# One-hot rows of the slot tables laid out two tiles side by side instead of eight, in a recurrence with two expert layers

## What is computed

```python
# x, f_logit: (2, 5056, 256); N = 10112 tokens, D = 256, E = 8 experts, F = 1024
f = lower_bound + (1 - lower_bound) * sigmoid(f_logit)
for t in range(S):
    h = f[:, t] * h + (1 - f[:, t]) * x[:, t];  y[:, t] = h
x = y.reshape(N, D)
# layer 0: router by cosine similarity over tau; layer 1: router by x @ w_gate
expert_idx = argmax(logits, axis=1)
gate_w = softmax(logits)[arange(N), expert_idx]
for e in range(E):
    mask = expert_idx == e
    out[mask] = gate_w[mask, None] * (relu(x[mask] @ w1[e]) @ w2[e])
```

## Time and profile before

| | |
|---|---|
| Median of 3 runs | 1358.53 us (1357.48 to 1358.74) |
| The profiled execution, its own time | 1355.69 us |
| Its span, first to last instruction | 1353.9 us |
| Busy: PE / PEld | 98% / 94% |
| Busy: DVE / ACT / POOL | 72% / 61% / 32% |
| Mean granted clock of PE | 0.984 |

### The profile page before, as it was taken

The page is one execution under the profiler, slowest core; times in us unless marked ns, Lnnn a source line. Parts: engine busy times, 40 slices in busy tenths (PEclk is TensorE's granted clock), DMA queues, the critical chain, the costliest instruction groups (busy, mean ns, idle before and its releaser), DMA issues.

```text
span 1353.9 us, 30681 instructions
## 1 busy us (share of the span) xinstructions
PE 1324.5 (98%) x10645; PEld 1266.2 (94%) x10645; DVE 974.0 (72%) x1471; ACT 825.6 (61%) x1390; POOL 427.3 (32%) x459
## 2 busy tenths in 40 slices
PE   7999989999999999999999999999999999999996
PEld 6995449999999999999999999899999999999996
DVE  5877337777777777789877789777777777777773
ACT  5775246666666666666656666556666666666662
POOL 5663012111111111123222243224444444444432
PEclk9998699999999999999999999999999999999998
DMA  7999528666677666679767667447666666666650
GB/s 272 334 319 307 2 91 293 215 227 213 221 230 231 213 226 214 220 235 164 235 212 221 232 194 229 157 156 233 221 214 222 229 222 203 222 226 224 219 179 1
DMA packets 205671, 287.00 MB, mean 212 GB/s; under 512 B 41270, under 2 KB 167876, under 8 KB 205604
## 3 DMA queue, kind: packets, MB, share of 16 engines
q1 hardware_dynamic: 192068, 250.90, 59.8%
q0 software_dynamic: 13536, 35.21, 7.8%
HBM read 252.59 MB, written 35.44 MB: 213 GB/s over the span
## 4 chain that ended last, share of the span: by engine, by line
PE 93%; DVE 3%; ACT 1%; POOL 1%; issue 1%; DMA 0%; DVEq 0%; SPq 0%; ACTq 0%; POOLq 0%
PE bank L1522 39%; PE bank L1502 39%; PE bank L1426 4%; PE bank L1486 3%; PE bank L1402 2%; PE bank L1388 1%; PE bank L1367 1%; PE bank L1348 1%; PE bank L1361 1%; DVE hT L453 1%; DVE gx L443 1%; POOL fg L994 1%; DMA w1raw<-in_moe_w 0%; ACT th L1186 0%; ACT sq L1200 0%
## 5 line engine op out<-in xcount | busy, mean ns | idle before, releaser
L1502 PE MATMUL bank<-xs,w1h 128*128 128x256 f32 x3008 | 558.4, 283 | 3.0 <-DVE hl L743 1.5
L1502 PEld LDWEIGHTS bank<-xs,w1h 128*128 128x128 f32 x3008 | 460.7, 188 | 4.6 <-DVE hl L743 1.7
L1269 ACT ACTIVATE hh<-bank 128x512 fp32r<-128x512 f32 x376 | 224.6, 597 | 388.7 <-PE bank L1502 388.7
L1522 PE MATMUL bank<-w2h,hl 128*128 128x264 f32 (+1 forms) x1504 | 424.9, 282 | 0.0
L1522 PE MATMUL bank<-w2h,hh 128*128 128x264 f32 (+1 forms) x1504 | 424.9, 282 | 0.0
L1522 PE MATMUL bank<-w2l,hh 128*128 128x264 f32 (+1 forms) x1504 | 424.6, 282 | 0.0
L1502 PE MATMUL bank<-xs,w1l 128*128 128x256 f32 x1504 | 419.9, 279 | 0.0
L743 DVE SCALAR_TENSOR_TENSOR hl<-bank,hh 128x512 fp32r<-128x512 f32 x376 | 259.9, 691 | 189.0 <-ACT hh L1269 185.1
L1522 PEld LDWEIGHTS bank<-w2l,hh 128*128 128x128 f32 x1504 | 283.3, 188 | 0.0
L1522 PEld LDWEIGHTS bank<-w2h,hh 128*128 128x128 f32 x1504 | 283.2, 188 | 0.0
L1522 PEld LDWEIGHTS bank<-w2h,hl 128*128 128x128 f32 x1504 | 282.9, 188 | 0.0
(11 more groups left out here) (172 smaller groups left out, 960.4 us busy)
## 6 DMA issues: line engine op xcount, KB each, us to landing
w1raw<-in_moe_w SPq DMA_DIRECT2D x94, 1024.0 KB
w2raw<-in_moe_w SPq DMA_DIRECT2D x94, 1024.0 KB, 5.6
rows_b<-yb SPq DMA_DIRECT2D x94, 128.0 KB, 2.2
xin<-in_x SPq DMA_DIRECT2D x19, 512.0 KB, 5.2
fin<-in_f_logit SPq DMA_DIRECT2D x19, 512.0 KB, 7.0
rows_a<-h_rows SPq DMA_DIRECT2D x19, 512.0 KB, 5.3
w_stage<-in_moe_w SPq DMA_DIRECT2D x12, 512.0 KB, 7.9
xb<-rows_a,row_i POOLq DMA_INDIRECT x94, 4.9
```

The lines of the kernel that those rows point to most:

```text
L1269: nc.scalar.activation(hh[:, j, :], bank[j % UB][:, :], ACT.Relu).then_inc(hid_hi, 1)
L1502: ins = mm(bank[j % UB][:, f * GW:(f + 1) * GW], w[p][:, o:o + P], xs[:, p, a, c * GW:(c + 1) * GW], start=k == 0, stop=k == 3 * DC - 1)
L1522: ins = mm(bank[Y_BANK + rows_slot(i, t)][:, 0:n], a[:, j, f * GW + t * P:f * GW + (t + 1) * P], w[p][:, 2 * j + f, 0:n], start=(j, f, k) ...
```

## The change

`lane_oh`, `tile_oh` and `vals` get the layout [partition, chunk slot, pair of tiles, lane or slot tile, 2]: two tiles lie side by side instead of eight, and the four pairs of a chunk follow each other. TensorE reads both operands with a step of two elements, 4 bytes. The tables of numbers are repeated twice instead of eight times, and read again for each pair. VectorE's three operations now have rows of two elements innermost. Where a chunk has an odd number of tiles (the last of table 0, seven) the row is filled up; the column of `where` behind the last tile gets -1 from a GpSimd memset, for which VectorE's wait on `rep_ok` goes from 2 to 3. The number of instructions of each engine in a chunk stays, and so do the orders of work.

```diff
+        RH = RC // 2
-        lane_oh = sb("lane_oh", [P, RS, P, RC], bf16, sr)
-        tile_oh = sb("tile_oh", [P, RS, ST, RC], bf16, sr)
-        vals = sb("vals", [P, RS, 2 * ST, RC], bf16, sr)
+        lane_oh = sb("lane_oh", [P, RS, RH, P, 2], bf16, sr)
+        tile_oh = sb("tile_oh", [P, RS, RH, ST, 2], bf16, sr)
+        vals = sb("vals", [P, RS, RH, 2 * ST, 2], bf16, sr)
...
-        lane_rep = sb("lane_rep", [P, P, RC], bf16, sr)
-        tile_rep = sb("tile_rep", [P, ST, RC], bf16, sr)
+        lane_rep = sb("lane_rep", [P, P, 2], bf16, sr)
+        tile_rep = sb("tile_rep", [P, ST, 2], bf16, sr)
...
-                dve.wait_ge(rep_ok, 2)
+                dve.wait_ge(rep_ok, 3)
...
-                v.tensor_tensor(tile_oh[:, g % RS, 0:W, 0:w], tile_rep[:, 0:W, 0:w],
-                                where[:, 0, t0:t0 + w].unsqueeze(1).to_broadcast([P, W, w]),
-                                ALU.is_equal).then_inc(oh_ok, 1)
-                v.tensor_tensor(lane_oh[:, g % RS, :, 0:w], lane_rep[:, :, 0:w],
-                                where[:, 1, t0:t0 + w].unsqueeze(1).to_broadcast([P, P, w]),
-                                ALU.is_equal).then_inc(lane_ok, 1)
+                h = -(-w // 2)
+                def of_two(ap2, n):
+                    return ap2.rearrange("p (h r) -> p h r", r=2).unsqueeze(2).to_broadcast([P, h, n, 2])
+                v.tensor_tensor(tile_oh[:, g % RS, 0:h, 0:W, :],
+                                tile_rep[:, 0:W, :].unsqueeze(1).to_broadcast([P, h, W, 2]),
+                                of_two(where[:, 0, t0:t0 + 2 * h], W), ALU.is_equal).then_inc(oh_ok, 1)
+                v.tensor_tensor(lane_oh[:, g % RS, 0:h, :, :],
+                                lane_rep[:, :, :].unsqueeze(1).to_broadcast([P, h, P, 2]),
+                                of_two(where[:, 1, t0:t0 + 2 * h], P), ALU.is_equal).then_inc(lane_ok, 1)
                 dve.wait_ge(oh_ok, g + 1)
-                v.tensor_tensor(vals[:, g % RS, 0:W, 0:w], tile_oh[:, g % RS, 0:W, 0:w],
-                                tileno[:, t0:t0 + w].unsqueeze(1).to_broadcast([P, W, w]),
-                                ALU.mult).then_inc(valt_ok, 1)
+                v.tensor_tensor(vals[:, g % RS, 0:h, 0:W, :], tile_oh[:, g % RS, 0:h, 0:W, :],
+                                of_two(tileno[:, t0:t0 + 2 * h], W), ALU.mult).then_inc(valt_ok, 1)
...
-                    pool.iota(table[:, :, :], pattern=[[1, count_t], [0, RC]], base=0,
+                    pool.iota(table[:, :, :], pattern=[[1, count_t], [0, 2]], base=0,
...
+                pool.memset(where[:, :, TT:TT + 1], -1.0).then_inc(rep_ok, 1)
...
-                nc.scalar.activation(vals[:, g % RS, W:2 * W, 0:w], tile_oh[:, g % RS, 0:W, 0:w],
+                h = -(-w // 2)
+                nc.scalar.activation(vals[:, g % RS, 0:h, W:2 * W, :], tile_oh[:, g % RS, 0:h, 0:W, :],
                                      ACT.Copy, scale=part1[:, 0:1]).then_inc(valp_ok, 1)
...
-                    ins = mm(table, lane_oh[:, g % RS, :, t], vals[:, g % RS, 0:2 * W, t],
+                    ins = mm(table, lane_oh[:, g % RS, t // 2, :, t % 2],
+                             vals[:, g % RS, t // 2, 0:2 * W, t % 2],
                              start=first and t == 0, stop=last and t == w - 1)
```

## The result

| | before | after |
|---|---|---|
| Median | 1358.01 us (1356.64 to 1358.74) | 1315.51 us (1315.29 to 1316.71) |
| The profiled execution | 1355.69 us | 1315.59 us |
| Its span | 1353.9 us | 1313.8 us |
| Mean granted clock | 0.984 | 0.993 |

The ratio is 0.969 (95% interval 0.9677 to 0.9702): 42.5 us faster. The forecast was 36.3 us and 1322; the result lies 1.5 us under 1317, the low end of the range given. The two profiled executions differ by 40.1 us, the rest is that the one of before was a quick one of its kind, so 40.1 is what can be laid out by place.

A forecast was written before the change was run, and what follows sets the result against it. TensorE was taken to bound the kernel, 91% of the span. Gains of 23.0 (table 0) + 13.0 - 1.4 (table 2) + 1.7 (table 1) = 36.3 us, off the median 1358.53, gave 1322.2; range 1317 to 1332.

The forecast's parts named there:

- the step isn't the cause: Rival: L1426 is slow for another reason, TensorE keeps 0.34 and 0.231 us, time 1358.5; 3%.
- The walk: Table 0 followed chunk by chunk through TensorE, VectorE and ScalarE: stage ends at 150.1, not 173.16, 23.0 us earlier.
- The clock's rival: Rival: TensorE's clock still falls in table 0, gate steps 6.5 us longer, gain 28, time 1330.2; 6%.
- I take the middle, 0.093, for all three widths: TensorE's new pace at L1426: 0.093 us a matmul with 188, 124 or 64 columns, between 0.08 and 0.106.
- The upper bound, 0.106: TensorE's slowest expected pace, from sixteen eight-column matmuls in 1.69 us, each loading 128 fp32 weights 4 bytes apart.
- the 256-column row: Up block's twelve fp32r matmuls in 1.42 us: 256 columns 4 bytes apart take 0.118 us, 0.46 ns a column.
- the 1.7 of the sum: Table 1's term: 64 matmuls going from 0.120 to 0.093 us, 1.7 us gained.
- the lower bound of 0.08: TensorE's fastest expected pace, 0.08 us, from a bf16 matmul with 188 columns at a step of 2 bytes.
- a stretch in which VectorE was near full: From 832, VectorE busy 13.20 of 14.00, loads idle 0.69 us; charged to table 2's four steps, 1.4 us taken.
- the cliff I gave 7%: Rival: VectorE falls to one element a cycle on rows of two, time 1341.6; 7%.
- The slower rival: Rival: VectorE walks short rows one by one, 5 ns a place, table 0 20 us late, time 1402; 3%.
- the forecast's best case of 39.9: Sum of the three tables' gains at 0.08 us a matmul and no stall: 23.1 + 14.2 + 2.6 us.

The follow-up runs named there:

- weights_only: Against the kernel before, only the weights (lane_oh) get pairs side by side, tile_oh and vals keep eight; 1354.43 us, ratio 0.9982.
- moving_only: Against the kernel before, only the moving operand (tile_oh and vals) gets pairs side by side, the weights keep a step of 16 bytes; 1319.8 us.
- four_side: Against the changed kernel, four tiles side by side in place of two, a step of 8 bytes for both operands; 1323.81 us.
- lag: The changed kernel with TensorE's chunks of tables 1 and 2 one tick later than VectorE's; 1311.82 us.
- one_side: Against the changed kernel, one tile by itself, both TensorE operands contiguous, VectorE's innermost rows of one element; 1340.65 us.

## Why the prediction was off, point by point

- **The mechanism was right.** TensorE's table matmuls were slow for the step of their operands and for nothing else (`weights_only`, `moving_only`, `four_side`); the rival "the step isn't the cause" is out.
- **Table 0: right in kind and size.** 23.5 us against 23.0. The walk gave chunks 0 to 5 at VectorE's pace, 6 to 8 at ScalarE's, the end at 150.1; with the start 0.8 earlier it came at 148.8. The pace that was wrong below is worth 0.7 us at most on the 79 matmuls here (0.093 less 0.084 each), and the waits for VectorE and ScalarE hid a part of it. The clock's rival didn't happen (its 6.5 us for three gate steps should have been 7.1 by its own rows, 15.7 less 3 x 2.89). L556 (now L557) waits 3.35 us, foretold as about 4.
- **The step that failed: "I take the middle, 0.093, for all three widths, since the narrow ones would be held by the load."** Measured: 0.084 for 188 columns, 0.056 for 124 and 0.030 for 64. The upper bound, 0.106, came from a load of 128 fp32 weights; a bf16 load isn't like it, it takes 0.060 even at 16 bytes (`moving_only`) and 0.030 or less at 4. I had the moving pace, 0.46 ns a column, in hand from the 256-column row: by it alone table 1 comes to 0.029 and table 2 to 0.057. Table 1 gave 5.3 us, three times the 1.7 of the sum and twice its best bound of 2.6, since the lower bound of 0.08 was itself for 188 columns and couldn't bound 64.
- **Table 2: two errors that partly cancel, so that 11.6 against 10.8 is in part luck.** TensorE's own step is 13.28 (`lag`) and not 13.8; over the table its matmuls alone were worth 15.4 us (80.33 less 64.96) and not 13.0. But the loop over three engines took 1.2 us a step (14.46 against 13.28), and not 0.35: I had charged the idle time of a stretch in which VectorE was near full, and no wait of one engine for the next in a circle. The step came to 14.46, foretold 14.2. The step in which the first chunk falls, where the chain runs over VectorE's preparation of the table, gave 0.6 us back; I had nothing there.
- **VectorE's rows of two: right.** 684 and 544 ns. `one_side` shows that the cliff I gave 7% is real and lies one step further, at 25 us.
- **The slower rival** had the right threshold question and the wrong price: rows cost nothing down to two elements, and rows of one cost 1.2 ns an element (1218 / 1024), not 5.
- **The range.** The profiles' 40.1 us is a shade outside the forecast's best case of 39.9, 0.8 of it ahead of the table, where no edit was made and where the profiles here differ by some 2 us. The other 2.4 us to 42.5 is the choice of base: the profiled execution of before was quicker than its median, that of after wasn't.

## What to carry to other kernels

Read the pace of a matmul against its columns, and where it is far over the best row of the same engine, look at the bytes between elements of each operand: the moving operand cost in proportion to its step here, from 4 bytes up, and the weights showed only when columns were few. Choose the layout so that the writer still gets two bf16 elements side by side; that was worth 42 us here, and one step further either way lost 8 or 25. When a slow engine is freed, look at the new waits in the chain: a consumer one tick behind its producer gave another 3.7 us for one number changed.

## What was not expected of the hardware

- The moving read of bf16 took 0.45 ns a column at 4 bytes, 0.92 at 8 and 1.8 at 16 (124 columns); contiguous is hardly quicker than 4 bytes (0.054 against 0.056 us). At 16 bytes it took the same 0.34 us for 188 columns at a granted clock of 1.00 and of 0.50.
- A load of 128 bf16 weights takes 0.060 us at a step of 16 bytes, and no more than 0.030 at 4 or 2; the fp32 load that I took for its like shows 0.106.
- In the changed kernel table 0's gate steps ran at 1.00 of the clock throughout. In `one_side`, where TensorE waited long for VectorE's rows (busy 4.98 of the 7.00 us from 137 to 144), it was 0.55 there.
